# Storing the folded weights from SyncE, placing the last stage's quarters earlier, and making the second unit's factors later, in a one-core two-MoE kernel

## The reference, cut to what matters

```python
kv  = einsum('bhsd,bhse->bhde', k, v)              # 8 batches, 8 heads, 576 tokens, 64 wide
x   = einsum('bhsd,bhde->bhse', q, kv)             # then RMS norm times g_norm
x   = (1 / (1 + exp(-(x @ w_gate)))) * (x @ w_val) @ w_out      # 4608 x 512, 1536 wide inside
h   = x @ w_in                                     # 2048 wide
g   = where(h >= 1, h, where(h <= -1, 0, (h + 1) ** 2 / 4))
out = g @ w_out                                    # 4608 x 512, all in float32
```

## Time and profile before

| | us |
|---|---|
| three runs | 1757.97, 1762.51, 1758.91; median 1758.91 |
| the profiled execution | 1760.77, with a span of 1759.0 inside it |
| PE busy | 1680.4 (96%), mean granted clock 0.981 |
| DVE, ACT, POOL busy | 1215.1, 886.3, 227.4 |

### The profile page before, as it was taken

One profiled execution on the slowest core, in us unless ns is written; L12 is line 12 of the kernel. 1 busy time (PEld: TensorE's weight loads), 2 busy tenths in 40 slices (PEclk: granted clock), 3 DMA queues, 4 the chain that ended last, 5 costly groups with the idle time before them and its releaser, 6 DMA issues. The chain is left out here.

```text
span 1759.0 us, 31916 instructions
## 1 busy us (share of the span) xinstructions
PE 1680.4 (96%) x12552; PEld 1641.2 (93%) x12552; DVE 1215.1 (69%) x1725; ACT 886.3 (50%) x1612; POOL 227.4 (13%) x293
## 2 busy tenths in 40 slices
PE   8999999999879999899999899999995799999999
PEld 5799999999879999899999899999995799999999
DVE  4567677678657775787778777777773576667764
ACT  5556666655435554444445455555552344444443
POOL 3510000014333442100002500000001100000000
PEclk9999999999989999999999999999997999999999
DMA  7444443333777788944533423333338944434440
GB/s 255 136 144 132 143 145 128 104 127 126 196 198 217 211 238 258 301 142 147 151 131 137 142 104 129 130 130 130 135 135 276 304 140 128 125 120 145 143 121 37
DMA packets 229316, 278.90 MB, mean 159 GB/s; under 512 B 33072, under 2 KB 172848, under 8 KB 229168
## 3 DMA queue, kind: packets, MB, share of 16 engines
q1 hardware_dynamic: 191568, 207.66, 36.0%
q0 software_dynamic: 37600, 69.22, 13.4%
HBM read 156.76 MB, written 120.06 MB: 157 GB/s over the span
## 5 line engine op out<-in xcount | busy, mean ns | idle before, releaser
L1500 PE MATMUL x<-t_hi,v_lo 128*128 128x288 f32 x1664 | 501.3, 301 | 34.7 <-ACT kept L877 19.0
L1501 PE MATMUL x<-t_lo,v_hi 128*128 128x288 f32 x1664 | 495.2, 298 | 0.0
L1502 PE MATMUL x<-t_hi,v_hi 128*128 128x288 f32 x1664 | 494.0, 297 | 0.0
L1500 PEld LDWEIGHTS x<-t_hi,v_lo 128*128 128x128 f32 x1664 | 316.1, 190 | 42.1 <-ACT kept L877 21.2
L1502 PEld LDWEIGHTS x<-t_hi,v_hi 128*128 128x128 f32 x1664 | 317.3, 191 | 0.0
L1501 PEld LDWEIGHTS x<-t_lo,v_hi 128*128 128x128 f32 x1664 | 316.7, 190 | 0.1
L1500 PE MATMUL y<-t_hi,v_lo 128*128 128x288 f32 x832 | 250.9, 302 | 26.3 <-DVE c_tile L1054 19.6
L1501 PE MATMUL y<-t_lo,v_hi 128*128 128x288 f32 x832 | 247.5, 297 | 0.0
L1502 PE MATMUL y<-t_hi,v_hi 128*128 128x288 f32 x832 | 246.7, 296 | 0.0
L1500 PEld LDWEIGHTS y<-t_hi,v_lo 128*128 128x128 f32 x832 | 158.1, 190 | 32.5 <-DVE c_tile L1054 20.0
L1500 PE MATMUL x<-v_hi,t_lo 128*128 128x256 f32 x576 | 164.2, 285 | 8.7 <-ACT o_kept L1021 8.7
(11 more groups left out here) (195 smaller groups left out, 3647.4 us busy)
## 6 DMA issues: line engine op xcount, KB each, us to landing
g_scratch<-c_tile SPq DMA_DIRECT2D x128, 288.0 KB, 2.4
gq<-g_scratch SPq DMA_DIRECT2D x64, 512.0 KB, 6.2
h_scratch<-gate SPq DMA_DIRECT2D x192, 144.0 KB, 2.1
hq<-h_scratch SPq DMA_DIRECT2D x32, 864.0 KB, 5.1
stage<-w_in POOLq DMA_DIRECT2D x68, 256.0 KB, 3.3
kv_ring<-kv_in SPq DMA_DIRECT2D x30, 512.0 KB, 4.4
fold_hi<-fold_hi POOLq DMA_DIRECT2D x14, 896.0 KB, 5.4
fold_lo<-stage POOLq DMA_DIRECT2D x14, 896.0 KB, 7.4
```

The costliest lines, as they stand in the source:

```text
L1500: nc.tensor.matmul(dst, s_lo, m_hi, start=start, stop=False, skip_group_check=True)
L1501: nc.tensor.matmul(dst, s_hi, m_lo, start=False, stop=False, skip_group_check=True)
L1502: return nc.tensor.matmul(dst, s_hi, m_hi, start=False, stop=stop, skip_group_check=True)
```

## The change

1. SP stores each fold, the high part right behind ACT's split and the low part right behind DVE's, in the step in which it is made. POOL no longer stores; it waits that fold `task - 1` has landed, and loads on. `load_b(0)` and `load_b(1)` come one task earlier. The scratch tensors are float32 now, seen as float32r where they are read.
2. `hq` quarters of block 0 are loaded in steps 88, 90, 92, 94 (0, 3, 1, 2) instead of 92 to 95 (0, 1, 3, 2).
3. Weight tasks 9 and 11 are split one step earlier (46, 50). The split of task 1 on DVE comes ahead of three operations on data factors. Tasks 30 and 31 are split in steps 0 and 1 of stage C instead of at the end of stage B, and tasks 32 and 33 in steps 3 and 4 instead of 1 and 2.
4. The `gq` quarters lie elsewhere. Unit 0 gets three of them in the sixth block of C and one at the start of the last; unit 1 gets two in the last block and two behind the last step, as before.
5. In unit 0 of stage D, the factors of unit 1 are made behind the products 7, 3 and 4 and not from product 6 on (`made_after`).

```diff
-SECOND_SETS = {40: 0, 43: 1, 45: 2, 47: 3, 49: 4, 51: 5}
+SECOND_SETS = {40: 0, 43: 1, 45: 2, 46: 3, 49: 4, 50: 5}
+THIRD_SETS = {0: 4, 1: 5, 3: 6, 4: 7}
...
+        def made_after(u, j):
+            if u == 0:
+                return ((5,), (6,), (), (), (7,), (8, 9), (10, 11))[j]
+            return range(SEVEN * u + j + D_SLOTS, min(SEVEN * u + j + D_SLOTS + 1, SEVEN * UNITS))
...
+            def store_fold_hi(task):
+                sp.wait_ge(v_hi_done, task + 1)
+                sp.dma_start(fold_place(task, 0), fold_hi[:].bitcast(f32)).then_inc(fold_stored[task % 2], 16)
+
+            def store_fold_lo(task):
+                sp.wait_ge(v_ready, task + 1)
+                sp.dma_start(fold_place(task, 1), stage[:, task % 2, :, :]).then_inc(fold_stored[task % 2], 16)
...
                 if k:
                     store_h0(k - 1)
+                if k in FOLDS:
+                    store_fold_hi(FOLD1_TASK + FOLDS[k])
...
+                if k in FOLDS:
+                    store_fold_lo(FOLD1_TASK + FOLDS[k])
+                if k == A_STEPS - 8:
                     all_stored(sp, h0_stored, k, 16)
                     all_stored(sp, h1_stored, k, 16)
+                    load_quarter_h(0)
...
                 else:
-                    all_stored(sp, g_stored, C_STEPS - C_SETS, 32)
+                    load_quarter(0, 1)
                 for s in range(C_SETS):
-                    if b == C_BLOCKS - 1 and s < 6:
-                        load_quarter(s // 4, (2, 3, 0, 1, 2, 3)[s])
+                    if b == C_BLOCKS - 3 and s == 0:
+                        sp.wait_ge(v_ready, TASKS)
+                        all_stored(sp, g_stored, C_SETS * b, 32)
+                    if b == C_BLOCKS - 3 and s in (0, 2, 4):
+                        load_quarter(0, (2, 3, 0)[s // 2])
+                    elif b == C_BLOCKS - 1 and s in (2, 5):
+                        load_quarter(1, (2, 3)[s // 3])
                     store_hidden(C_SETS * b + s)
...
                 if is_fold(task - 1):
-                    store_fold(task - 1)
-                    if task == C_TASK:
-                        for i in range(B_LOADS):
-                            load_b(i)
-                    else:
-                        fold_is_stored(task - 1)
+                    fold_is_stored(task - 1)
                 elif 0 < task < TASKS - 1:
                     pool.wait_ge(v_ready, task)
+                if task == C_TASK - 1:
+                    load_b(0)
+                    load_b(1)
+                elif task == C_TASK:
+                    for i in range(2, B_LOADS):
+                        load_b(i)
...
-                if 1 <= k < 3:
-                    split_weights(C_TASK + 5 + k)
+                if k in THIRD_SETS:
+                    split_weights(C_TASK + THIRD_SETS[k])
```

More of the change, by code:

```diff
@@ L91, in program @@
     g_dram = scratch("g_scratch", [S2, P, TOK])
-    fold1_dram = [scratch(f"fold1_{part}", [SEVEN, P, J1, CHUNK], f32r) for part in ("hi", "lo")]
-    fold2_dram = [scratch(f"fold2_{part}", [SEVEN, P, J2, CHUNK], f32r) for part in ("hi", "lo")]
+    fold1_dram = [scratch(f"fold1_{part}", [SEVEN, P, J1, CHUNK]) for part in ("hi", "lo")]
+    fold2_dram = [scratch(f"fold2_{part}", [SEVEN, P, J2, CHUNK]) for part in ("hi", "lo")]
     ctx = ExitStack()
@@ L167, in program @@
         c_kept = place("c_kept", O + 36864, [P, 4, C])
-        gq = [[place(f"gq0{x}", O + 4096 * x, [P, J2, ROWS]) for x in range(4)],
-              [place(f"gq1{x}", O + at, [P, J2, ROWS]) for x, at in enumerate((23040, 27648, 45696, 49792))]]
-        s_sum = place("s_sum", O + 41600, [P, J2, ROWS])
+        gq = [[place(f"gq{u}{x}", O + at, [P, J2, ROWS]) for x, at in enumerate(places)]
+              for u, places in enumerate(((41600, 0, 45696, 49792), (23040, 27648, 8192, 12288)))]
+        s_sum = place("s_sum", O + 4096, [P, J2, ROWS])
         o_tile = [place(f"o_tile{i}", O + at, [P, 2, DM]) for i, at in enumerate((16384, 31744))]
@@ L422, in _, with fold_place, load_quarter_h @@
             store_x(0, 1)
+            def fold_place(task, part):
+                if task < FOLD2_TASK:
+                    return fold1_dram[part][:, :, task - FOLD1_TASK, :].rearrange("x p n -> p x n")
+                return fold2_dram[part][:, :, task - FOLD2_TASK, :].rearrange("x p n -> p x n")
+            def store_fold_hi(task):
[4 more added lines that the diff above has]
+                sp.dma_start(fold_place(task, 1), stage[:, task % 2, :, :]).then_inc(fold_stored[task % 2], 16)
+            def load_quarter_h(x):
+                sp.dma_start(hq[x][:], h_dram[J1 * (x // 2):J1 * (x // 2 + 1), :, C * (x % 2):C * (x % 2 + 1)]
+                             .rearrange("j p n -> p j n")).then_inc(hq_loaded[x], 16)
             for k in range(A_STEPS + 1):
@@ L622, in sum_right @@
                 nc.gpsimd.tensor_tensor(st[6], st[2], st[5], ALU.subtract).then_inc(stage_summed, 1)
[L624 to L627, removed]
-                    j = task - (FOLD1_TASK if task < FOLD2_TASK else FOLD2_TASK)
-                    pool.dma_start(dram[:, :, j, :].rearrange("x p n -> p x n"), part).then_inc(fold_stored[task % 2], 16)
             def fold_is_stored(task):
@@ L636, in load_factor @@
                     for base, at, count in pieces:
-                        pool.dma_start(ring[:, base:base + count, :], dram[quad, :, first + at:first + at + count, :]).then_inc(loaded, 16)
+                        pool.dma_start(ring[:, base:base + count, :], dram[quad, :, first + at:first + at + count, :].bitcast(f32r)).then_inc(loaded, 16)
             def load_b(i):
@@ L642, in load_b @@
                     for parity in range(2):
[L643 removed]
+                        fold_is_stored(C_TASK - 4 + parity)
                 elif 2 <= i < 4:
@@ L1042, in _ @@
                         nc.scalar.copy(o_tile[u % 2][:, 1, 0:R], X[u % 2][:, 0:R]).then_inc(c21_ready, 1)
-                    e = SEVEN * u + j + D_SLOTS
-                    if e < SEVEN * UNITS:
+                    for e in made_after(u, j):
                         split_d_item(e)
@@ L1330, in _ @@
                 if k == 0:
+                    split_weights(1)
                     sum_item(0, 5)
@@ L1455, in _ @@
                     split_c_item(b + 1, 2)
-                if k < 3:
-                    split_weights(C_TASK + 5 + k)
+                if k in THIRD_SETS:
+                    split_weights(C_TASK + THIRD_SETS[k])
                 if k == C_STEPS - 1:
@@ L1481, in _ @@
                         add(o[:, 0, R:], Y[u % 2][:, 0:R], o_kept[:, 2, :]).then_inc(c12_ready, 1)
-                    nu, i = divmod(SEVEN * u + j + D_SLOTS, SEVEN)
-                    if nu < UNITS:
+                    for e in made_after(u, j):
+                        nu, i = divmod(e, SEVEN)
                         if nu > u:
```

19 lines of the change are left out of this document (7 added, 12 removed).

## The result

The changed kernel takes **1719.26 us** (median of four runs, 1718.49 to 1721.21) against 1759.06 for the kernel before in the same session: a ratio of 0.9772, 95% interval 0.9755 to 0.9789. It is 40 us faster; 66 were forecast, and 1719 lies above the range of 1680 to 1712. Its profiled execution has a span of 1717.6 us, 41.4 less than the 1759.0 of before.

The account below looks back on a forecast made before the run. The prediction took PE's own work plus its losses at a few places to bound the kernel. Gains of 22 + 2.5 + 4.5 + 11.5 + 24 + 1.5 = 66 us gave 1693 us, range 1680 to 1712.

Parts of the forecast that it names:

- From C to D: gain 24: Stage C's end into D: quarters loaded earlier and unit 0 finishing meanwhile let unit 1 start sooner; gain 24 us, 17 to 29.
- the rival of the last wait: Ahead of unit 1: its 512-byte pieces behind 4 KB factor loads still take 16 us; gain 12, time 1705, chance 0.16.
- For the later stretch: gain 2.5: Steps 69 to 94: the fold's low part lands about 1 us sooner; gain 2.5 us, 0 to 4.5.
- Past SP's queue: cost 0: SP's queue: hidden stores behind fold stores still land within the 8 us they have before DVE rewrites their place; cost 0.
- End of stage A: 4.5: Step 94 to stage B: the wait of 4.76 us goes, with loads and quarters earlier; gain 4.5 us, 2 to 6.
- Start of C: 11.5: Stage C's first steps: PE's three waits go, as weight splits and task 33's sums are moved; gain 11.5 us, 7 to 12.
- Folds: gain 22: Steps 53 to 69, six folds: SP's earlier stores remove most waits for the fold, leaving 6 us lost; gain 22, 17 to 24.5.
- The rival by which another issuer saves only issuing time: First six folds: moving the stores saves only POOL's issue of two stores, 2 us a fold; 12 us in all.
- Start: 1.5: Task 1: its low part, split ahead of DVE's data operations, shortens PE's wait of 3.67 us; gain 1.5, 0 to 2.8.
- bytes bind: Folds and last block of C: DMA bytes bind, halving both gains to 11 and 12; time 1716, chance 0.12.
- Only the last wait stays: C to D: unit 1's quarters take 16 us after the backlog, so it starts near 1400; gain 12, time 1705, chance 0.16.
- Slower: All 14 fold steps: DVE waits for hidden stores behind the fold stores, at 6.5 us a fold; time 1776, chance 0.03.

Follow-up runs that it names:

- paired: The change with neighbouring stage D quarters loaded as pairs in 1 KB pieces, at other places, unit 1's ahead of step 63's store: 1710.16 us, 0.9717 to before.
- quarters_behind: The change with quarters 2 and 3 of unit 1 moved from steps 58 and 61 to behind stage C's last step: 1711.88 us, 0.9729 to before.
- half_packets: The change with POOL's factor loads of stage D in 2 KB packets for 4 KB, twice the issues, same bytes: 1716.48 us, 0.9754 to before.
- old_end: The change with stage A's end as before: all factor loads in task 26, the four quarters in steps 92 to 95: 1716.72 us, 0.9775 to before.
- b_loads_late: The change with all seven of POOL's stage B factor loads in task 26 again, none in task 25: 1728.56 us, 0.9812 to before.
- one_load_early: The change with only the first stage B factor load in task 25 and the second in task 26: 1720.84 us, 0.9795 to before.
- b_small_packets: The change with POOL's stage B factor loads in 2 KB packets for 6 KB, three times the issues, same bytes: 1721.64 us, 0.9785 to before.
- folds_alone: The kernel before with only SP's two fold stores in place of POOL's, nothing else of the change: 1740.34 us, 0.9891 to before.

## Why the prediction was wrong

**"From C to D: gain 24"** is the step that failed first, by 11.2 us. Its frame was one pool of bytes at 347 GB/s, in which a transfer lands when the bytes ahead of it are through. Two of its parts held: no wait of DVE for `gq` in steps 60 to 63 is left, and the last wait of PE ahead of unit 1 is 2.6 us. Stage D was to start 23.2 us sooner, less what the stores hold; measured from the copy of step 5 of C it starts 8.7 sooner (at 1343.53), and 18.2 sooner in paired, where DVE's waits for `g_scratch` in the block are 2.25 and 0.46 us. What failed stands in the prediction's last sentence on it: "If the stores of `g_scratch` hold steps 61 to 63, up to 5 are lost". They did, for 9.18 us and a fall of the clock (0.60 in the window from 1320 to 1330), 10.1 us in sum by quarters_behind. half_packets shows why. While both queues have work, SP's moves one packet for each of POOL's, so a quarter of 1024 packets of 512 bytes costs the time of 1024 packets of 4 KB, some 11 us at 382 GB/s (an estimate), and the stores stand behind it. The change left two quarters of unit 1 in the block where POOL's queue is never empty, the first of them two steps earlier than before, and the prediction priced them by their 1.05 MB; by packets they were the dearest thing in the queue. I named the size of the pieces, 512 bytes, in the rival of the last wait, and did not carry it to the stores.

**"For the later stretch: gain 2.5"** and **"Past SP's queue: cost 0"** failed together, by 7.9. The price for a hidden store behind a low part, 2 + 2.6 + 1 us for 8 to be had, nearly held in the thirteen earlier folds, where DVE waits 2.3 us for `h_scratch` in all. It failed at the last, the one fold beside which the same change issues two factor loads. These I had counted only where they left, as 9 us less at the end of stage A, and not where they arrived. The new places of the loads and of the `hq` quarters together cost more than they bring, by the 4.8 us of old_end. Which of the transfers is late is chance of place (the fold's stores in the change, quarter 0 in b_loads_late and one_load_early); that 1.6 to 3.1 MB of loads and 0.9 to 1.8 MB of SP's start together ahead of a hidden store is common to all. That bytes, not packets, set the end there is shown for the fold's stores (one_load_early against b_small_packets); for quarter 0 it is argued from them.

The 2.5 itself was wrong too: folds_alone moves the eight later folds by 0.1. Every second one still waits for `fold_lo`, 0.75 to 2.47 us in its profile. The DMA carries 237 GB/s there before and 239 after; whether the bytes or the chain of load, sums and store sets this rest was not tried.

**"End of stage A: 4.5"** was 3.0: the wait of 4.76 became 1.41 at 689.55, not the none that was named as its sign. **"Start of C: 11.5"** was 9.8: the mechanism held, and by the windows some 2 us went to the two small holes.

**"Folds: gain 22"** was right, 19.8 in the change and 18.3 in folds_alone, though single profiles of one stretch spread by 8. The six folds lose 8.3 us where I took 6 (its own terms, 2, 2, 1.4 and 1.4, make 6.8), in the places named (the pairs of steps with a load of `xo`): 2.9 and 3.7 for the 2 each. The rival by which another issuer saves only issuing time gave 12; folds_alone is 6 above it, and the least of the fourteen other kernels with these instructions, 15.2, 3 above. So the gain came mostly of something else than issuing time: the store leaves earlier, and on another queue, which were not tried apart. **"Start: 1.5"** came as forecast, but the kernels with this start reach step 53 at 435.8 to 438.5 us and the two without it at 438.0 and 438.9, so a single profile does not show it. The order of `made_after` was worth about 5.

Of the rivals, the time of "bytes bind", 1716, is nearest to the result, but not its mechanism. "Only the last wait stays" gave the right size for C to D, 12, at the wrong place: it is the wait that all but went. "Slower" had the right object, hidden stores behind fold stores, and came true, above 2 us, behind one fold of fourteen.

## What to carry to other kernels

Price a transfer on a queue in packets as well as in bytes wherever another queue is never empty: the DMA view of any such stretch (here 906 to 904) tells what a packet waits for. Before a load is moved earlier, list what is issued in the ten microseconds around its new place, and which small store with a reader stands behind it in the same queue. Where two executions of the same instructions differ by 8 us in one stretch, as the folds do here, read an edit from its own stretch.

## What the runs showed of the hardware

- Two queues with work moved equal numbers of packets, at three mixes of sizes: 906 to 904 (before, 1340 to 1350), 724 to 722 (the change, 1312 to 1320), 1089 to 1083 (half_packets, 1310 to 1318). Alone, with packets of some 1 KB, SP's queue moved 1140 in three microseconds (the change, 655 to 658).
- It did not hold from the first microsecond. SP's store of a fold part was issued at 643.06, between POOL's loads, and in 644 to 646 POOL's queue moved 136 packets and SP's none; from 648 to 652 it was 237 to 237. The quarter issued at 1303.24 shows the same: 144 packets to none from 1304 to 1306. What sets the delay was not tried.
- An issue can take long: SP's store at 648.05 took 5.83 us to issue, where 0.32 is usual, with both parts of the fold (1.8 MB) issued ahead of it and not landed. What holds it was not tried.
